# Odd keys of the first four jobs turned by GpSimd, and their state increments issued behind the second tile of the feed-forward stage

## The reference

```python
# attention part: B=4, H=8, S=768, D=48
f = sigmoid(f_logit)
for t in range(S):
    state = f[:, :, t, :, None] * state + k[:, :, t] (outer) v[:, :, t]
    y[:, :, t] = q[:, :, t] @ state
x = y as (B*S, H*D) = (3072, 384)
# first feed-forward part, d_ff = 2048
h = x @ w_in;  x = (max(h, 0) ** 2) @ w_out
# second feed-forward part, same sizes
h = x @ w_in2; out = (h * tanh(softplus(h))) @ w_out2
```

## Time and profile before

| | us |
|---|---|
| median of 3 runs (885.55 to 886.59) | 885.93 |
| the profiled execution | 886.69 |
| its span | 885.0 |
| PE busy | 874.3 (99%) |
| DVE busy | 597.2 (67%) |
| ACT busy | 594.8 (67%) |
| GpSimd busy | 62.0 (7%) |

### The profile page before, as it was taken

The page is one execution under the profiler, slowest core; times in us unless marked ns, Lnnn a source line. Parts: engine busy times, 40 slices in busy tenths (PEclk is TensorE's granted clock), DMA queues, the critical chain, the costliest instruction groups (busy, mean ns, idle before and its releaser), DMA issues.

```text
span 885.0 us, 16260 instructions
## 1 busy us (share of the span) xinstructions
PE 874.3 (99%) x6282; PEld 725.3 (82%) x6282; DVE 597.2 (67%) x1054; ACT 594.8 (67%) x1026; POOL 62.0 (7%) x71
## 2 busy tenths in 40 slices
PE   8899999999999999999999999999999999999998
PEld 7788888888888888888788888888888888888886
DVE  6879545445544444342244799999898898898886
ACT  6776655564546555544566787888887887877874
POOL 0222111111111111110000000000000000000000
PEclk9999999999999999999999999999999999999999
DMA  9644221122212111100233201001001001000100
GB/s 255 203 148 128 76 81 44 44 81 65 66 45 80 44 44 57 46 13 1 92 96 100 90 19 37 37 0 37 37 1 37 36 1 37 36 0 1 36 1 36
DMA packets 25090, 50.64 MB, mean 57 GB/s; under 512 B 2674, under 2 KB 3442, under 8 KB 25010
## 3 DMA queue, kind: packets, MB, share of 16 engines
q1 hardware_dynamic: 25010, 49.56, 18.0%
HBM read 40.11 MB, written 9.44 MB: 56 GB/s over the span
## 4 chain that ended last, share of the span: by engine, by line
PE 98%; DMA 1%; issue 0%; SPq 0%; ACT 0%; DVE 0%; ACTq 0%
PE ps L1069 45%; PE ps L1086 44%; PE ps L1043 2%; PE ps L1013 2%; PE ps L1039 2%; PE ps L991 1%; PE ps L1059 1%; DMA work<-fkq 1%; SPq L284 0%; PE ps L988 0%; PE ps L997 0%; SPq L297 0%; ACT work L497 0%; ACT work L538 0%; SPq L306 0%
## 5 line engine op out<-in xcount | busy, mean ns | idle before, releaser
L1069 PE MATMUL ps<-xs,w_hi 128*128 128x512 f32 x1152 | 359.3, 393 | 1.0 <-issue 1.0
L1069 PEld LDWEIGHTS ps<-xs,w_hi 128*128 128x128 f32 x1152 | 213.0, 188 | 45.0 <-issue 1.6
L1086 PE MATMUL ps<-g_hi,w_lo 128*128 128x512 f32 x576 | 224.1, 389 | 0.0
L1069 PE MATMUL ps<-xs,w_lo 128*128 128x512 f32 x576 | 224.1, 389 | 0.0
L1086 PE MATMUL ps<-g_hi,w_hi 128*128 128x512 f32 x576 | 224.1, 389 | 0.0
L1086 PE MATMUL ps<-g_lo,w_hi 128*128 128x512 f32 x576 | 224.1, 389 | 0.0
L829 DVE TENSOR_TENSOR g_lo<-gb,g_hi 128x512 fp32r<-128x512 f32 x96 | 68.1, 709 | 215.6 <-ACT gb L564 215.6
L559 ACT ACTIVATE rb<-ps 128x512 f32<-128x512 f32 x96 | 57.3, 597 | 161.0 <-PE ps L1069 161.0
L1069 PEld LDWEIGHTS ps<-xs,w_lo 128*128 128x128 f32 x576 | 108.1, 188 | 22.6
L1086 PEld LDWEIGHTS ps<-g_hi,w_hi 128*128 128x128 f32 x576 | 108.1, 188 | 22.5
L1086 PEld LDWEIGHTS ps<-g_hi,w_lo 128*128 128x128 f32 x576 | 108.1, 188 | 22.4
(11 more groups left out here) (82 smaller groups left out, 750.6 us busy)
## 6 DMA issues: line engine op xcount, KB each, us to landing
work<-fkq SPq DMA_DIRECT2D x68, 224.0 KB, 3.7
stage<-w SPq DMA_DIRECT2D x24, 384.0 KB, 3.1
work<-v_tok SPq DMA_DIRECT2D x22, 256.0 KB, 3.9
x_scratch<-yo SPq DMA_DIRECT2D x6, 768.0 KB, 3.8
xs<-x_scratch SPq DMA_DIRECT2D x6, 768.0 KB, 4.4
out<-work SPq DMA_DIRECT2D x17, 256.0 KB, 2.1
yo<-w SPq DMA_DIRECT2D x8, 384.0 KB, 4.6
work<-f_tok SPq DMA_DIRECT2D x4, 224.0 KB, 3.5
```

Of the source, the lines that this page charges most:

```text
L1069: ins = nc.tensor.matmul(bank, w[:, f, k * P:(k + 1) * P], xs[:, half, part, k, :], start=k == 0 and i == 0, stop=k == KT - 1 and i == 2)
L1086: ins = nc.tensor.matmul(ps[:, 5 + d, :], w[:, f, cols], g[:, slot, :], start=f == 0 and i == 0, stop=f == NF - 1 and i == 2)
```

## The change

- `keys(j)` for j < 4 issues four transposes. For the odd pairs it reads `turned`, a copy with the halves exchanged, made by GpSimd in two copies a job (`turn`), and waits for `kt_turned` ahead of pair 1. `turned` lies in `rb`, one buffer for all four jobs, so `turn(j)` waits for the transposes of job j - 1.
- The transposed keys of jobs 2 and 3 go to `eb` and no longer to the buffer of jobs 0 and 1. So `keys_out` of jobs 2 and 3 no longer waits for increments, and stands earlier in ACT's list, while `inverse_decay(4)` and `(5)`, which write `eb`, now wait for the increments of jobs 2 and 3.
- The increments of jobs 0 to 3 are two matmuls a head pair in place of four, and PE issues all of them in iteration 1, behind `up1(1)`. The second square of tiles 0 and 1 writes `gb`, where the values of jobs 2 and 3 lie, and so waits for these increments too.
- PE's list has the scores of a job ahead of the sums of a later one and of the transposes. ACT and DVE move the logarithm and cap of job 2 behind the growth of job 1 and the keys of job 0. `weights_lo(2)` moves ahead of `state(0)`.
- The products that nobody reads are two of 384 columns, and later one, in place of six and three of 128 columns.

```diff
-    IDLE = [6, 3]
+    IDLE = [(3, 3), (3,)]
...
+        turned = rb[:, C:C + 2 * C].rearrange("p (n h t) -> p n h t", n=2, h=2)
...
         def key_rows(j):
+            if j in (2, 3):
+                return eb[:, j % 2, :, :].rearrange("p n t -> p (n t)")[:, 0:NP * R].rearrange("p (n r) -> p n r", r=R)
             return ktT[:, j % 2, :, :]
...
+            def turn(j):
+                pool.wait_ge(s_["kt_ready"], j + 1)
+                wait(pool, s_["kT_done"], j)
+                k = kt[0:R, j % 2, 1::2, :].rearrange("p n (h t) -> p n h t", h=2)
+                for h in range(2):
+                    nc.gpsimd.tensor_copy(turned[0:R, :, h, :], k[:, :, 1 - h, :]).then_inc(s_["kt_turned"], 1)
+            for j in range(B):
+                turn(j)
...
             def inverse_decay(j):
+                if j < B + 2:
+                    act.wait_ge(s_["kv_done"], j - 1)
...
             def keys_out(j):
-                elif j >= 2:
-                    act.wait_ge(s_["kv_done"], j - 1)
...
             def squares(t):
                 wait(act, s_["g1_ready"], t - 1)
+                if t < 2:
+                    act.wait_ge(s_["kv_done"], t + 3)
                 nc.scalar.activation(gb[:, t % 2, :], rb[:, :], ACT.Square).then_inc(s_["g1_raw"], 1)
...
             first_growth(0)
             first_decay(0)
-            first_logarithm(2)
             first_growth(1)
             first_decay(1)
+            first_logarithm(2)
...
             x1_hi(0)
+            keys_out(2)
             weights_hi(0)
             x1_hi(1)
+            keys_out(3)
...
             weights_hi(1)
-            keys_out(2)
-            keys_out(3)
             weights_hi(2)
             inverse_decay(4)
...
             first_cap(1)
-            first_cap(2)
             first_keys(0)
             first_queries(0)
+            first_cap(2)
...
             weights_lo(1)
+            weights_lo(2)
             state(0)
             state(1)
-            weights_lo(2)
...
                 for n in (0, 2, 1, 3):
+                    k = kt[0:R, j % 2, n, :]
                     if j < B and n % 2 == 1:
-                        for at in (0, HC):
-                            ins = nc.tensor.matmul(ps_k(j)[at:at + HC, n, :], kt[0:R, j % 2, n, HC - at:C - at], ident[0:R, 0:R],
-                                                   start=True, stop=True, skip_group_check=True, tile_position=(0, at))
-                    else:
-                        ins = nc.tensor.transpose(ps_k(j)[:, n, :], kt[0:R, j % 2, n, :], ident[0:R, 0:R])
+                        if n == 1:
+                            pe.wait_ge(s_["kt_turned"], 2 * j + 2)
+                        k = turned[0:R, n // 2, :, :].rearrange("p h t -> p (h t)")
+                    ins = nc.tensor.transpose(ps_k(j)[:, n, :], k, ident[0:R, 0:R])
...
+                parts = ROWS if j < B else [(Q * i, min(Q * i + Q, R)) for i in range(4)]
                 for n in range(NP):
-                    for i in range(4):
-                        lo, hi = Q * i, min(Q * i + Q, R)
-                        v0, v1 = VALUES[i // 2]
-                        ins = nc.tensor.matmul(ps_kv(j)[lo:hi, n, :], key_rows(j)[:, n, lo:hi], v_rows(j)[:, 2 * n + i // 2, v0:v1],
+                    for lo, hi in parts:
+                        v0, v1 = VALUES[lo // GAP]
+                        ins = nc.tensor.matmul(ps_kv(j)[lo:hi, n, :], key_rows(j)[:, n, lo:hi], v_rows(j)[:, 2 * n + lo // GAP, v0:v1],
                                                start=True, stop=True, skip_group_check=True, tile_position=(0, lo))
...
                     up2(t)
+                if k == 1:
+                    for j in range(B):
+                        increments(j)
                 for u in downs(k):
                     down1(u)
...
             idle_products(IDLE[1], 6)
+            scores(0)
             sums(2)
-            scores(0)
             keys(0)
+            scores(1)
             sums(3)
-            scores(1)
             keys(1)
             values(0)
+            scores(2)
             keys(2)
-            scores(2)
             values(1)
+            scores(3)
             keys(3)
-            scores(3)
-            increments(0)
             values(2)
             values(3)
-            increments(1)
-            increments(2)
-            increments(3)
             for k in range(SPLIT):
                 iteration(k)
```

More of the change, by code:

```diff
@@ L190, in attention_ffn @@
             ft_exped ft_capped ft_logged sums_done m_ready
-            exped inv_f scanned logged p_ready ends_kept kt_ready gp_ready qp_ready qt_ready pc_ready
+            exped inv_f scanned logged p_ready ends_kept kt_ready kt_turned gp_ready qp_ready qt_ready pc_ready
             kT_done kT_out a_done a_out y_done kv_done s_added s_ready
@@ L1143, in iteration, with idle_products @@
                     keys(j)
-            def idle_products(count, bank):
-                for i in range(count):
-                    nc.tensor.matmul(ps[:, bank, 0:P], ident[:, :], ident[:, :], start=True, stop=True, skip_group_check=True)
+            def idle_products(widths, bank):
+                for n in widths:
+                    nc.tensor.matmul(ps[:, bank, 0:n * P].rearrange("p (n t) -> p n t", t=P), ident[:, :],
+                                     ident[:, :].unsqueeze(1).to_broadcast([P, n, P]), start=True, stop=True, skip_group_check=True)
             pe.wait_ge(s_["const_ready"], 4)
```

## The result

The changed kernel takes 889.12 us (median of 9, 887.77 to 890.22), the old one 886.20 beside it: ratio 1.0032, interval 1.0023 to 1.0040, so 2.9 us slower. The forecast was 886.5, no measurable change, with 8 chances in 10 for 883.5 to 888.5. The profiled execution took 888.82 with a span of 887.1, 2.1 above the old span.

A forecast was written before the change was run, and what follows sets the result against it. PE, busy 874.3 of 885.0 us, was the bound: 4.6 earlier, 1.8 of carried increments, 3.4 of new idle time, so +0.6, 887.3 profiled, 886.5 for the median; range 885.3 to 887.7, 8 in 10 for 883.5 to 888.5.

The forecast's parts named there:

- the two tiles: PE's first two large tiles from the start of up1(0), forecast at 2.08 us each, 4.15 us together.
- the load chain: From the issue of v(4) on SP to the landing of weights 4: 7.8 us as before, setting the start of scores(4).
- The gaps are missing code: PE's "issue" gaps of 0.37 and 1.55 us before up1(0): PE ran out of code; none expected after the change.
- T = 24.05: Forecast start of up1(0), set by DVE's chain, 4.6 us earlier than the old 28.62.
- The 0.4 us for contention: GpSimd's turning copies beside DVE's queries 2 and 3, priced at 0.2 us each, delaying up1(0).
- Three engines wait behind T: ACT, DVE and SP wait for the late increments: PE idles 1.45, 0.6 and 1.3 us ahead of up1(2), down1(0), scores(4).
- The increments at 0.45 each: Each job's increments behind up1(1) take PE 0.45 us, so v(4) is issued 5.55 us behind the start of up1(0).
- Rival 4: PE's idling between 20 and 34 drops the clock to half, costing 2 us or more; chance 0.05 with the unforeseen.

The follow-up runs named there:

- s1: Changed kernel with the four increments directly behind values(3), ahead of up1(0), instead of behind up1(1): 884.32 us against the old kernel's 886.79, ratio 0.9972.
- s10: s6 with the increments of jobs 0 to 3 in four matmuls a pair again: 884.00 us, ratio 0.9973 to the old kernel.
- s12: Old kernel with five loads (f(4), weights 2, k(4), q(4), weights 3) issued only when values(1) is done: 888.93 us, ratio 1.0034.
- s6: s1 with the loads of q(4) and weights 3 issued only when values(3) is done: 883.36 us against the old kernel's 886.43, ratio 0.9964.
- s9: s6 with the turning undone: split matmuls on PE, no GpSimd copies: 883.94 us, ratio 0.9969 to the old kernel.
- s11: s6 with the load of weights 4 issued ahead of that of v(4): 883.47 us, ratio 0.9969 to the old kernel.
- s4: Changed kernel with squares(0) ahead of inverse_decay(4) on ACT: 888.87 us, ratio 1.0019 to the old kernel.
- s2: Changed kernel with two unread products of 384 columns behind values(3), filling PE's wait ahead of up1(0): 888.77 us, ratio 1.0021 to the old kernel.
- s5: Changed kernel run once more, unedited, as yardstick: 888.84 us, ratio 1.0024 to the old kernel.
- s3: Changed kernel with the load of weights 4 issued ahead of that of v(4): 887.39 us, ratio 0.9999 to the old kernel.
- s7: Changed kernel with increments behind up1(0), ahead of up1(1), and weights 4 loaded ahead of v(4): 885.29 us, ratio 0.9986 to the old kernel.
- s8: Changed kernel with the turning undone: split matmuls on PE, no GpSimd copies: 888.94 us, ratio 1.0028 to the old kernel.

## Why the prediction was wrong

Two terms of its sum failed: the two tiles, taken at full clock, and the load chain, taken at the old 7.8 us. A third part of the miss, lost at full clock too, stays open. Its steps one by one:

- **The gaps are missing code: shown.** In s1, s10 and s12 they stand at the places that the count of PE's instructions gives, each about 1.5 us behind the end of a code packet. That the loads make the packet late rests on the times of s6 and s9 to s11 against s1 and on the third gap of s12; the first gap of s12 did not follow them. That none would stand in the changed kernel was right.
- **T = 24.05: nearly right.** `up1(0)` started at 22.92, and at 23.40, 23.46 and 23.57 in s4, s2 and s5. DVE's chain was the limit, as said. The 0.4 us for contention did not appear. The chain began with keys 2 at 12.81 in place of the 13.79 of the forecast, which held them to the landing of their load; that is 0.98 of the 1.13 us. In s4 they began as early, at 12.79, but 0.5 of it was lost in a wait for `scores(3)` that the forecast put at nothing:

```profile
18.96 0.86 DVE L788 TENSOR_TENSOR work<-ps,causal 64x256 f32<-64x256 f32 x2 [0.59 <-PE ps L1031]
```

  PE was behind from the start there: the 16 matmuls of its first sums took 3.49 us, against 2.35 in the profile of the changed kernel.
- **Three engines wait behind T: right, and near in size.** Forecast 1.45, 0.6 and 1.3 us of idle time; measured 1.59, 0.26 and 1.66. s4 shows that ACT's head wait alone is worth nothing, s3 that the load chain is the last tie, s1 and s7 that the place of the increments is the cause of all three.
- **The increments at 0.45 each: low.** v(4) was issued 1.7 us behind the first increment's start where 1.4 were taken.
- **The load chain, "the same 7.8 us pass": mis-sized.** It took 8.2 (changed), 8.8 (s5), 8.0 (s2), 8.2 (s4) and 7.9 (s8). The chain ties one to one, so this is 0.1 to 1.0 us of the loss. In the first four, SP's issues from v(4) to weights 4 took 2.48, 2.68, 1.90 and 2.43 us, before 1.81; the rest of the way, from the issue of weights 4 to the landing, stayed at 5.7 to 6.1. Why single issues took up to 1.30 us in place of 0.43 is not shown.
- **The clock: the step that failed, for a part of the miss.** The sum has no term for it: "two tiles" stand at 4.15 us, at full clock. Rival 4 priced a fall at 2 us or more and was given 0.05 with the unforeseen, because gaps of 1.55 and 1.43 us had not brought one. But the clock fell in 11 of the 20 executions of the changed kernel, against 10 of 35, 9 of 33 and 3 of 22 of the old one. In the profile the two tiles took 5.88 us, and as the fall stands ahead of the increments, all of it goes down the load chain: T to v(4) was forecast at 5.55 and took 7.58.

In the profiled execution the sum goes: T 1.13 earlier than forecast, the two tiles 1.7 longer, the increments 0.3 longer, the landing 0.4 longer, which is 1.3 of the 1.46 by which `scores(4)` missed its forecast (2.06 against 0.6). That T came 1.13 us early there, and hid as much of the loss, was luck.

In the medians the clock is the smaller part or half. The kernel lost 2.9 us in the result and 2.4 in s5, where 0.6 were forecast. The falls account for 1.3 of the missing 2.3 in the result (889.12 less 887.84, the median of its three executions at full clock), and for 0.6 of the missing 1.8 in s5. The other 1.0 to 1.2 us are lost at full clock as well, and their cause stays open. The profiles at full clock show only a part: `scores(4)` missed its forecast by 0.2 (s2) and 0.3 us (s4). The landing was a whole us late in the profile of s5, and no run tells how often that comes; but s3, in which the landing is no tie, had as much missing at full clock.

Nor is it shown what brings a fall. The wait of 1.65 us ahead of `up1(0)` is not enough: the clock did not fall behind it in the profiles of s4, s5, s7 and s8, and s7 and s8 had a fall in 2 of 11 and 1 of 10 executions only. In all profiles with a fall it came behind an idle time of PE of 1.5 us or more (changed, s1, s3, s5, s12).

## What to carry to other kernels

Work moved out of an idle time to a later place frees the engine but delays every semaphore that it signals; follow each waiter's queue (the load queue too) before counting the gain. In stretches of many small matmuls under full DMA load, count instructions: code comes in packets over the DMA engines that carry the loads, and a gap called "issue" inside a run of equal instructions was such a packet here. Not every "issue" is one: ahead of `scores(4)` it stood for DVE's queries, so look which engine ended just before. Filling an engine's idle time with its own later work (s6) released the waiters, went with fewer falls of the clock, and shortened the way to `scores(4)`. And look at the single executions: a median can lie between two kinds (s1), and one profile shows one of them.

## What the runs showed of the hardware

- PE's code packets (16 KB) took from 2 to over 5 us from the end of a block, near 18, to their start, between 19.8 and 23.8, while the DMA engines carried about 265 GB/s, in profiles of the same start of the program (s1). PE went on about 1.5 us after a packet had ended (23.38 + 1.05 to 25.98 in s1, 21.78 + 1.23 to 24.57 in the old kernel). In the old trace that load of the DMA engines lasts to about 23 us, not to 25.
- A GpSimd copy of 112x128 elements takes 0.29 us (s2, `turn(2)`); beside DVE's queries and keys, which read two operands, the copies get longer, up to 1.19 for two, and the DVE steps by 0.08 at most (0.77 in s4, 0.76 in s11, against 0.69), where a GpSimd product of two operands had stretched a DVE product from 0.67 to 1.23.
- A job's increments in two parts of 64 columns a pair took 0.51 us, in four parts of 32 columns 0.39 (s6, s10): half the instructions, but not less time. The old kernel's rows of four parts had given 0.36 and 0.53.
- In the same start of the program the 16 matmuls of the first sums took 2.35 us in one profile and up to 3.55 in another (s2), 0.15 to 0.22 us each, where 8 of the next sums take 0.96, 0.12 each. The granted clock reads 1.00 in that stretch in both, so it does not show this difference; its cause is not shown.
